# Masked log weights in one matrix product, gate rows laid by DMA, in a fused attention and two MLP kernel

## What is computed

```python
for t in range(S):
    m_new = np.maximum(f_gate[:, :, t] + m, i_gate[:, :, t])
    f_stab = np.exp(f_gate[:, :, t] + m - m_new)
    i_stab = np.exp(i_gate[:, :, t] - m_new)
    C = f_stab * C + i_stab * np.einsum('bhd,bhe->bhde', vt, kt)
    n = f_stab * n + i_stab * kt
    y[:, :, t] = o * einsum(C, qt) / np.maximum(np.abs(einsum(n, qt)), 1.0)
x = attention output, tokens x 320
h = x @ w_in;  g = (a0 + a1 h + a2 h^2 + a3 h^3) / (1 + |b0||h| + |b1|h^2 + 1e-6);  x = g @ w_out
xn = x / rms(x) * rms_g;  out = (silu(xn @ w_gate) * (xn @ w_val)) @ w_out2
```

## Time and profile before

| | us |
|---|---|
| median of 3 runs | 471.13 |
| lowest, highest | 468.38, 481.77 |
| the profiled execution | 468.82 |
| its span | 467.0 |
| TensorE busy | 455.5 (98% of the span) |
| VectorE, ScalarE, GpSimd busy | 328.5, 289.4, 250.6 |
| chain that ended last: TensorE, VectorE, ScalarE | 82%, 5%, 3% of the span |

### The profile page before, as it was taken

One profiled execution on the slowest core, in us unless ns is written; L12 is line 12 of the kernel. 1 busy time (PEld: TensorE's weight loads), 2 busy tenths in 40 slices (PEclk: granted clock), 3 DMA queues, 4 the chain that ended last, 5 costly groups with the idle time before them and its releaser, 6 DMA issues.

```text
span 467.0 us, 7429 instructions
## 1 busy us (share of the span) xinstructions
PE 455.5 (98%) x2679; PEld 398.8 (85%) x2680; DVE 328.5 (70%) x462; ACT 289.4 (62%) x468; POOL 250.6 (54%) x271
## 2 busy tenths in 40 slices
PE   8999999988999999999999999999999999999997
PEld 4888997866999888998899888888888888888886
DVE  7999997998899998999999543484343444534333
ACT  6788887799889999999988648532111222211111
POOL 4476698858898897988989555981000000000000
PEclk9999999999999999999999999999999999999999
DMA  8998930230000000000005030000010000100001
GB/s 245 332 317 267 268 92 1 91 135 1 0 1 1 1 1 1 0 1 0 2 0 214 2 135 3 0 1 0 1 56 1 0 0 1 44 14 1 1 0 58
DMA packets 8372, 26.78 MB, mean 57 GB/s; under 512 B 1216, under 2 KB 3136, under 8 KB 7824
## 3 DMA queue, kind: packets, MB, share of 16 engines
q1 hardware_dynamic: 8336, 26.30, 17.6%
HBM read 24.33 MB, written 1.97 MB: 56 GB/s over the span
## 4 chain that ended last, share of the span: by engine, by line
PE 82%; DVE 5%; ACT 3%; issue 2%; POOL 1%; DVEq 0%; POOLq 0%; ACTq 0%
PE ps L1620 7%; PE ps L1621 7%; PE ps L1622 7%; PE ps L1550 6%; PE ps L1552 6%; PE ps L1551 6%; PE ps L1568 4%; PE ps L1569 4%; PE ps L1570 4%; PE ps L1528 4%; PE ps L1526 4%; PE ps L1527 4%; PE ps L1624 3%; PE ps L1625 3%; PE ps L1474 2%; PE ps L1529 2%
## 5 line engine op out<-in xcount | busy, mean ns | idle before, releaser
L992 ACT ACTIVATE ab<-ps 128x512 f32<-128x512 f32 x36 | 21.6, 599 | 117.6 <-PE ps L1625 117.6
L1337 DVE TENSOR_TENSOR ab<-ps,ab 128x512 f32<-128x512 f32 x36 | 24.9, 691 | 84.7 <-ACT ab L992 84.7
L589 POOL TENSOR_TENSOR qq<-qq,ab 128x512 f32<-128x512 f32 x48 | 61.2, 1296 | 20.9 <-ACT qq L836 20.8
L595 POOL TENSOR_TENSOR g_lo<-cc,g_hi 128x512 fp32r<-128x512 f32 x48 | 61.9, 1310 | 6.0 <-ACT g_hi L858 6.0
L1550 PE MATMUL ps<-wo_hi,g_hi 128*128 128x320 f32 x192 | 59.9, 312 | 2.1 <-POOL g_lo L595 1.1
L1552 PE MATMUL ps<-wo_hi,g_lo 128*128 128x320 f32 x192 | 59.3, 309 | 0.0
L1551 PE MATMUL ps<-wo_lo,g_hi 128*128 128x320 f32 x192 | 59.3, 309 | 0.0
L1568 PE MATMUL ps<-wo_hi,g_hi 128*128 128x320 f32 x136 | 42.0, 309 | 0.2 <-ACT g_hi L1000 0.2
L1570 PE MATMUL ps<-wo_hi,g_lo 128*128 128x320 f32 x136 | 42.0, 309 | 0.0
L1569 PE MATMUL ps<-wo_lo,g_hi 128*128 128x320 f32 x136 | 42.0, 309 | 0.0
L1550 PEld LDWEIGHTS ps<-wo_hi,g_hi 128*128 128x128 f32 x192 | 36.0, 188 | 5.7 <-issue 2.6
(11 more groups left out here) (189 smaller groups left out, 1252.5 us busy)
## 6 DMA issues: line engine op xcount, KB each, us to landing
qk<-q_k_dram SPq DMA_DIRECT2D x12, 448.0 KB, 9.0
wo_raw<-w_out_dram SPq DMA_DIRECT2D x7, 640.0 KB, 7.0
kv<-kv_n_dram SPq DMA_DIRECT2D x10, 372.0 KB, 6.9
w_raw<-w_main_dram SPq DMA_DIRECT2D x4, 512.0 KB, 7.7
out_dram<-y_out SPq DMA_DIRECT2D x12, 160.0 KB, 1.9
w2c_raw<-w_main_dram SPq DMA_DIRECT2D x1, 1536.0 KB, 6.2
sig_o<-o_n_dram SPq DMA_DIRECT2D x1, 1280.0 KB, 7.7
rest_raw<-w_rest_dram SPq DMA_DIRECT2D x2, 512.0 KB, 7.6
```

The source lines that it names most:

```text
L589: pool.tensor_tensor(qq[m % 2][:, h, :], qq[m % 2][:, h, :], ab[m % 2][:, h, :], ALU.mult)\
L595: pool.tensor_tensor(glo(n), cc[n // 2 % CR][:, n % 2, :], ghi(n).bitcast(F32), ALU.subtract)\
```

## The change

From iteration 5 on (`FOLD`) the mask product is left out. Rows 64 to 127 of the product's two operands now form the mask: the new gBm holds in them, twice over, a mask for the lower and for the upper 64 queries of a chunk, and sel holds in them a one-hot pattern of the query within its half. It is written once for each batch: by `one_hot_first` on VectorE, where `spread_whole(5)` stood, and by `one_hot_second` on ScalarE. The two products of an iteration are no longer one for each four heads, but one for each half of the queries with all eight heads; ScalarE's exponential puts the halves together through its access pattern. The values A of the chunk go into rows 16 (rounded) and 17 (remainder) of sel, against ones in gBm: two DMAs of 4 KB each, from SBUF to SBUF, in ScalarE's queue (`rows(it)`), two iterations or more ahead of their product. `spread` stays for iterations 2 to 4.

b for the chunks 2 to 5 is laid into gBm twice (once for each half): ScalarE's copy in `gate_rows_b` and GpSimd's remainder `low_of_halves` in iterations 2 (256 columns) and 3 (768 columns). GpSimd's split_main1(0) moves from iteration 3 to 4, split_main1(1) from 4 to 5, where split_rest1(0) stands already. It also forms the half masks in the prologue, and gB's memsets are halved. gif moves to another place, so that b is not overwritten.

The gate columns become transposes. TensorE gets products with zeros, of 512 columns: one ahead of scores(2), two behind it, one ahead of intra(2).

```diff
             def gate_rows_b(i):
+                part = slice(SEG[i].start, 3 * L)
                 act.wait_ge(b_done, i + 1)
-                act.activation(gB[0:BH, SEG[i]], i_g[:, SEG[i]], ACT.Copy).then_inc(b_hi, 1)
+                act.activation(gB[0:BH, part], i_g[:, part], ACT.Copy).then_inc(b_hi, 1)
+                shape = [BH, 2, S - 2 * L]
+                act.activation(gBm[0:BH, :, :], i_g[:, 2 * L:].unsqueeze(1).to_broadcast(shape), ACT.Copy).then_inc(m_hi, 1)
+            def masks():
+                act.wait_ge(mask_ready, 1)
+                shape = [P - 64, 2, NC - 2, P]
+                act.activation(gBm[64:P, :, :].rearrange("p f (c l) -> p f c l", l=L),
+                               mask_h[64:P, :, :].unsqueeze(2).to_broadcast(shape), ACT.Copy).then_inc(masked, 1)
+            def one_hot_second():
+                act.wait_ge(d_done, 4)
+                act.activation(sel[64:P, H:BH, :].rearrange("p h (f l) -> p (h f) l", l=Q2),
+                               ident[64:P, 64:P].unsqueeze(1).to_broadcast([P - 64, 2 * H, Q2]), ACT.Copy).then_inc(onehot[1], 1)
+            def rows(it):
+                c, b = divmod(it, B)
+                act.wait_ge(d_done, it - B + 1)
+                act.wait_ge(rounded_consts, b + 1)
+                act.wait_ge(low_a_done, 2)
+                heads, tokens = slice(b * H, (b + 1) * H), slice(c * L, (c + 1) * L)
+                act.dma_start(sel[16:17, heads, :].bitcast(F32), gA[b * H:(b + 1) * H, tokens].bitcast(F32)).then_inc(rows_in[b], 16)
+                act.dma_start(sel[17:18, heads, :].bitcast(F32), gA[32 + b * H:32 + (b + 1) * H, tokens].bitcast(F32))\
+                    .then_inc(rows_in[b], 16)
...
-                if it < NT - B and it + 2 != ON_DVE:
+                if it + 2 < FOLD:
                     spread(it + 2)
+                elif it + 3 < NT:
+                    rows(it + 3)
                 if it == 1:
+                    masks()
                     gate_rows_a(1)
                 if it == 2:
                     columns(1)
+                    rows(FOLD)
+                    one_hot_second()
...
-                if it == 3:
+                if it == 2:
+                    low_of_halves(2, 3, 1)
+                elif it == 3:
+                    low_of_halves(3, NC, 2)
+                elif it == 4:
                     split_main1(0)
-                elif it == 4:
+                elif it == 5:
                     split_main1(1)
-                elif it == 5:
                     split_rest1(0)
...
+            def one_hot_first():
+                dve.wait_ge(consts, 2)
+                dve.wait_ge(d_done, FOLD)
+                dve.tensor_copy(sel[64:P, 0:H, :].rearrange("p h (f l) -> p (h f) l", l=Q2),
+                                ident[64:P, 64:P].unsqueeze(1).to_broadcast([P - 64, 2 * H, Q2])).then_inc(onehot[0], 1)
...
-                    mm = pe.matmul(ps[:, 7, at_:at_ + BH], cumA[:, c * L:(c + 1) * L], ident[0:BH, 0:BH],
-                                   start=True, stop=True)
+                    mm = pe.transpose(ps[:, 7, at_:at_ + BH], cumA[:, c * L:(c + 1) * L], ident[0:BH, 0:BH])
...
+            def log_weights_masked(it):
+                c, b = divmod(it, B)
+                pe.wait_ge(exp_done, it)
+                pe.wait_ge(low_m_done, min(c - 1, 2))
+                pe.wait_ge(masked, 1)
+                pe.wait_ge(onehot[b], 1)
+                pe.wait_ge(rows_in[b], 32 * ((it - FOLD) // B + 1))
+                for f in range(2):
+                    mm = pe.matmul(psDh[f], gBm[:, f, (c - 2) * L:(c - 1) * L], sel[:, b * H:(b + 1) * H, f * Q2:(f + 1) * Q2],
+                                   start=True, stop=True)
+                mm.then_inc(d_done, 1)
...
+                if it == 2:
+                    warm_up(1, 5)
                 for h in range(H):
                     mm = pe.matmul(psO[:, h, :], E[it % 2][:, h, :], v1[r][:, h, :], start=True, stop=True)
...
             for it in range(1, NT - 2):
-                if it >= 2:
+                if it + 1 >= FOLD:
+                    log_weights_masked(it + 1)
+                elif it >= 2:
                     causal(it + 1)
                     log_weights(it + 1)
+                if it == 1:
+                    warm_up(1, 6)
+                if it >= 2:
                     carry(it)
...
                 if it >= 3:
                     transposes(it - 3)
+                if it == 1:
+                    warm_up(2, 6)
                 intra(it)
                 updates(it)
-            causal(NT - 1)
-            log_weights(NT - 1)
+            log_weights_masked(NT - 1)
```

More of the change, by code:

```diff
@@ L42 @@
 EARLY = (7, 8, 9, 10, 11, 17, 18, 19, 20, 21, 22, 24)
-ON_DVE = 5
+FOLD = 5
+Q2 = L // 2
 WARM = 14
@@ L204, in build @@
         psD_all = ps[:, 2:4, :].rearrange("p b (h l) -> p (b h) l", **heads)
+        psDh = [ps[:, 2 + f, :].rearrange("p (h l) -> p h l", l=Q2) for f in range(2)]
+        psDh_all = ps[:, 2:4, :].rearrange("p f (h l) -> p h f l", l=Q2)
         psD1 = [ps[:, 5 + i, :].rearrange("p (h l) -> p h l", **heads) for i in range(2)]
@@ L288, in build @@
         low_b_done = sem("low_b_done")
+        low_m_done = sem("low_m_done")
+        m_hi = sem("m_hi")
+        mask_ready = sem("mask_ready")
+        rows_in = [sem(f"rows_in{b}") for b in range(B)]
+        masked = sem("masked")
+        onehot = [sem(f"onehot{b}") for b in range(B)]
         ends_ready = sem("ends_ready")
@@ L475, in _ @@
             pool.nop().then_inc(consts, 1)
+            pool.memset(gBm[0:64, :, :].bitcast(F32), 1.0)
+            own(pool.memset(mask_h[:, :, :], 0.0))
+            pool.affine_select(out=mask_h[:, :, :], in_=mask_h[:, :, :], compare_op=ALU.is_ge, fill=NEG, base=-64,
+                               pattern=[[Q2, 2], [-1, P]], channel_multiplier=1).then_inc(mask_ready, 1)
+            pool.wait_ge(mask_ready, 1)
             def input_steps(i):
@@ L496, in low_of_b, with low_of_halves @@
                 pool.wait_ge(low_b_done, i + 1)
+            def low_of_halves(c0, c1, done):
+                part = slice((c0 - 2) * L, (c1 - 2) * L)
+                b = i_g[:, c0 * L:c1 * L].unsqueeze(1).to_broadcast([BH, 2, (c1 - c0) * L])
+                pool.wait_ge(m_hi, 1)
+                pool.tensor_tensor(gBm[32:32 + BH, :, part], b, gBm[0:BH, :, part].bitcast(F32), ALU.subtract)\
+                    .then_inc(low_m_done, 1)
+                pool.wait_ge(low_m_done, done)
             def ones(it):
@@ L1100, in spread_whole @@
                 dve.wait_ge(rounded_consts, b + 1)
[L1101 to L1104, removed]
+                dve.wait_ge(low_a_done, 1)
+                dve.tensor_tensor(sel[64:P, mine, :], gA[:, 0:L].bitcast(F32).unsqueeze(1).to_broadcast(shape),
                                   sel[0:64, mine, 0:1].bitcast(F32).to_broadcast(shape), ALU.mult).then_inc(whole_spread, 1)
+            def one_hot_first():
[3 more added lines that the diff above has]
+                                ident[64:P, 64:P].unsqueeze(1).to_broadcast([P - 64, 2 * H, Q2])).then_inc(onehot[0], 1)
             gate_maxima(0)
```

24 lines of the change are left out of this document (13 added, 11 removed).

## The result

The changed kernel takes 494.63 us (median of 4 runs, 491.87 to 500.8); the kernel before, beside it, 471.62 us. The ratio is 1.048, with a 95% interval of 1.043 to 1.054: 23 us slower. The profiled execution took 500.8 us, with a span of 498.9.

The account below looks back on a forecast made before the run. TensorE looked like the bound, VectorE having hardly any slack and GpSimd's chain from 56.16 us capping later gains at 0.73 us. +0.1 at wo_lo and −0.4 behind that chain gave 468.8 − 0.3 = 468.5 us, range 465 to 472.5.

Parts of the forecast that it names:

- the case of a fall of the granted clock: In TensorE's new wait at 36.5: one iteration at half rate, +5.4 us, 474; chance 0.02.
- The wait itself: Iteration 4, ahead of transposes(1): TensorE arrives early and waits 1.5 to 2.6 us for x_lo(0).
- 3.9 us of work: TensorE, iterations 4 to 10: seven mask pairs go, 0.55 us each, so TensorE has 3.9 us less.
- One-hot copy and den: VectorE, iterations 3 and 4: copy waits for low_of_halves till 35.1, gain zero; den's second step waits behind yo, 0.7 us later.
- the bounds of 0 to 0.7 us: ScalarE's cost of issuing one gate-row transfer, two per iteration: taken as 0.4 us, between nothing and 0.7.
- less late than forecast: ScalarE: x_hi(0) moves from 35.51 to about 36.9 through copies and issues, just hidden before VectorE wants it at 37.7.
- The landing of the gate rows: Row transfers cost nothing; the rival had them late, TensorE losing 3 us once and up to 1 in six iterations: 477, chance 0.03.
- The cap of GpSimd's chain: From wo_lo at 56.16 to 78.85 GpSimd runs without a real gap, so later TensorE gains pass on at most 0.73 us.
- The sum: Whole kernel: +0.1 − 0.4 = −0.3 us, from 468.8 to 468.5 us.
- +0.1: VectorE's wo_lo, after iterations 4 to 6, ends near 56.1, 0.1 us later than before (55.98).
- 0.4 of 0.73 us won: GpSimd's wait behind its chain: 0.73 us won if den slips ahead of w_st, otherwise 0.1; taken as 0.4.
- Case B: TensorE stays the bound to the end, some 4 us won: 464.8; chance 0.20.

Follow-up runs that it names:

- b_nomask: The kernel before without the mask products from iteration 5 on, the mask missing from the computation there; 497.4 us.
- a_zero: The changed kernel with two 512-column zero products ahead of the value products of iterations 4 to 9; 499.5 us, lowest 469.2.
- a_pro: The changed kernel with GpSimd's three half-mask instructions moved behind its first copy of b into gB; 480.0 us.
- a_adj: The changed kernel with two zero products directly ahead of each pair of masked log-weight products, where the mask products stood; 478.7 us.
- c_mask: The changed kernel with half masks behind the first copy of b, one-hot copy behind x_lo(0), and mask products kept but overwritten; 467.9 us.
- a_both: The changed kernel with half masks moved behind the first copy of b and the one-hot copy behind x_lo(0); 474.5 us.
- a_mask: The changed kernel with the mask products kept in their old place, overwritten by the masked log weights; 476.9 us.
- b_wait1: The kernel before with VectorE writing sel for iteration 5 twice, so that TensorE waits longer; 479.4 us.
- c_adj: The changed kernel with half masks behind the first copy of b, one-hot copy behind x_lo(0), zero products in the mask products' place; 467.9 us.
- b_nomask_wait1: The kernel before with sel for iteration 5 written twice and without the mask products from iteration 5 on; 500.6 us.

## Why the prediction was wrong

**The clock.** This is the step that failed: the case of a fall of the granted clock, to which the prediction gave a chance of 0.02 and a price of one iteration at half rate, 5.4 us. The wait itself was forecast (2.6 us at 36.5, and 1.5 to 2.6 us as a sign to look for; measured 2.45 at 43.37). In the forecast it was costed by its length alone. The chance was too small: all four runs fell, and with a wait of 2.18 us the kernel before has 18 to 25 us at half in all four runs (0.974 to 0.981), which only 2 of the 19 runs beside it reach. The price was wrong by a factor of five: 60 us at half rate and 29 us of loss, because the mask products were counted as 3.9 us of work and nothing else. b_nomask shows that their absence alone turns 472 us into 497. Behind what the changed kernel's three other runs fell is not known, since the wait of 2.45 us hangs on a race; that they stayed down some 60 us is in their mean clock.

**The prologue.** The prediction left out what GpSimd's three instructions for the half masks do to its copy of b. They delay the first log weights by 0.8 us (9.56 against 8.76) and lengthen a wait of TensorE, behind which the clock fell for 13.7 us in the profiled run, but not in the other three.

**One-hot copy and den.** Right where low_of_halves comes first. The copy was then stretched to 2.15 us (forecast: over 2), den to 1.08 us behind yo (forecast 0.67 for its second step; it was the first, and it met C as well). What the prediction left out is the race: in three of five profiled runs a late load of kv put low_of_halves behind the copy, which took 0.69 to 1.17 us. The Trainium skill's rule (SBUF — State Buffer, "SBUF: two separate sides") was applied to an instruction that no trace had shown yet, and held.

**ScalarE.** An issue of 0.63 us was inside the bounds of 0 to 0.7 us, but two of them delayed ScalarE by 0.37 us, not by 0.8. Nothing hung on it in the changed kernel's profile: x_hi(0) was there 2.2 us ahead of x_lo(0). Where the copy ran free it did: x_lo(0) waited 0.82 us for x_hi(0) in a_zero and 0.84 us in a_pro. Even so x_hi(0) was less late than forecast, 35.98 in a_zero against 36.9 (35.51 before).

**The landing of the gate rows.** Right: no wait of TensorE in any of these profiles ends with a row transfer.

**The cap of GpSimd's chain.** Right while the clock stays: a chain of 22.7 us, and 0.7 us to be won behind it. (In the changed kernel, at half clock, it is 34.9 us: 73.93 to 108.85.) The sum can only be held against kernels that are near the changed one, as no run of that itself kept its clock: with zero products it took 469.17 us (a_zero) and 468.68 us (a_adj) in runs with a clock of 1.00; forecast 468.5. That this is so near is partly luck. In a_zero's profile VectorE's wo_lo ended at 55.27, 0.7 us earlier than before, where the sum has +0.1; and GpSimd's wait behind its chain was 0.89 us, where the sum has 0.4 of 0.73 us won. Case B, TensorE as the bound, is refuted by c_mask.

**Still open.** What makes the clock fall. a_both fell behind a wait of 0.99 us and a_mask behind 0.76, b_wait1 and b_nomask also with no wait near, while the kernel before kept its clock behind 0.97 us at sel and behind 1.14 and 1.16 us at 108.9 and 113.9 us, among the wide products of the MLP. The runs give no limit. c_adj and c_mask, with waits of 0.5 to 0.7 us in the profiles, have a clock of 1.00 in six of eight runs and 0.995 and 0.996 in the other two, some 4 us at half. Nor do four wide products in a row always end a fall at once: in the changed kernel's first one six stand in a row from 12.7 to 15.6 us, and the clock is back at 24.6. It also wasn't tried how much of the 1 us between the kernel before and c_mask at full clock comes from ScalarE's saved spreads. And the kernel before falls a little in many of its runs (clock 0.99), which is most of c_adj's 1% lead; filling its own wait for sel wasn't tried.

## What to carry to other kernels

Cost a new wait of TensorE by what the granted clock does behind it, and not by its length: a wait of 2 to 3 us cost about 8 us where two pairs of 512 columns followed in the next iteration, and 26 to 28 us where they did not. Before taking products away because they carry little, look at what stands around them: in the profiles, from iteration 4 to the attention's end, the clock came back only behind two such pairs in a row. A wait seen in one profile can hang on which of two engines comes first, here by when a load lands; look at it in several. And when an engine that seems to be the bound gets less to do, look first for the chain that starts late and has no idle time; here GpSimd's, which let about 1 us through.

## What the runs showed of the hardware

TensorE can be busy without a gap in the profile (20.00 of 20.00 us in a_both and in b_nomask_wait1, stretch behind stretch) and yet stay at 1.2 GHz to the end of the attention. The Trainium skill (TensorE: Matmul & The Clock Gate, "Part 1: The HAM clock gate") has the full clock return once the engine has been kept busy again. By the busy time of the profile that is not what these stretches show: b_nomask_wait1 has 60 us of it and no return, b_wait1 has its return 13 us behind the wait.

The same two products with zeros brought the clock back when they stood next to the log weights (a_adj: at half for about 7 us in the profile, 31 and 34 us in all in its two slowest runs) and not when they stood some 3 us away from them (a_zero: 65 us and more in three of four runs). Their place counted and not their number.

The clock can also fall while TensorE is busy without a gap: in b_wait1 at 27.8 us, 9 us behind its last idle time.

A transfer of 4 KB from SBUF to SBUF took ScalarE's queue 0.63 us to issue, beside the instruction ahead of it; two of them held the next one up by 0.37 us.
